# Products of 64 rows in two row tiles, layer 2 eleven units behind, and the split of x moved to ScalarE and GpSimd

## The reference, cut to what matters

```python
# x (2, 4096, 192), weight (8 heads, 7 taps)
w = softmax(weight)                          # over the taps
x = causal_convolution(x, w)                 # 7 taps, one set for 24 channels; 8192 tokens of 192
h = x @ w_in1                                # 192 -> 2048
P = a[0] + a[1]*h + a[2]*h*h + a[3]*h*h*h
Q = 1.0 + abs(b[0])*abs(h) + abs(b[1])*h*h
x = (P / (Q + 1e-6)) @ w_out1                # 2048 -> 192
h = x @ w_in2                                # 192 -> 2048
return (s * maximum(h, 0)**2 + b2) @ w_out2  # 2048 -> 192
```

## Time and profile before

| | us |
|---|---|
| median of 3 runs | 1260.81 (1260.74 to 1261.53) |
| the profiled execution, its own time | 1262.06 |
| its span, first to last instruction | 1260.3 |
| PE busy in the span | 1250.0 |
| DVE busy | 1118.3 |
| ACT busy | 1073.5 |
| POOL busy | 327.9 |

### The profile page before, as it was taken

How to read it: one execution, slowest core, us unless ns; L and a number is a source line. 1 busy time by engine, 2 the same in 40 slices (tenths; PEclk the granted TensorE clock), 3 DMA queues, 4 the chain that set the end, 5 groups by cost and what they waited for, 6 DMA issues and landing times.

```text
span 1260.3 us, 16271 instructions
## 1 busy us (share of the span) xinstructions
PE 1250.0 (99%) x6018; PEld 1078.5 (86%) x6018; DVE 1118.3 (89%) x1029; ACT 1073.5 (85%) x1093; POOL 327.9 (26%) x152
## 2 busy tenths in 40 slices
PE   8999999999999999999999999999999999999999
PEld 5768888888888888888888888888888888888888
DVE  7998999998999989998999989999899998889750
ACT  6998888888889898898888889898898888888853
POOL 3443222223223223222222222222222232232200
PEclk9999999999999999999999999999999999999999
DMA  8100000010000100000000100001000000000000
GB/s 230 56 13 13 1 14 1 5 34 0 12 0 12 25 0 12 0 12 25 12 0 0 38 0 12 0 0 38 0 12 0 12 0 1 13 1 13 1 13 13
DMA packets 14748, 20.39 MB, mean 16 GB/s; under 512 B 1792, under 2 KB 9984, under 8 KB 14592
## 3 DMA queue, kind: packets, MB, share of 16 engines
q1 hardware_dynamic: 14576, 20.01, 5.6%
q10 hardware_dynamic: 144, 0.01, 0.0%
HBM read 13.72 MB, written 6.29 MB: 16 GB/s over the span
## 4 chain that ended last, share of the span: by engine, by line
PE 97%; DMA 1%; DVE 0%; SPq 0%; ACT 0%; POOL 0%; issue 0%
PE o L466 26%; PE h L448 5%; PE h L449 5%; PE h L417 5%; PE o L438 5%; PE o_tail L439 5%; PE o_tail L432 5%; PE o L430 5%; PE o L431 5%; PE h L459 5%; PE h L453 5%; PE h L458 5%; PE h L418 5%; PE h L419 5%; PE h L420 5%; PE h L421 5%
## 5 line engine op out<-in xcount | busy, mean ns | idle before, releaser
L406 POOL TENSOR_TENSOR gl<-work,gh 128x1024 fp32r<-128x1024 f32 x126 | 304.6, 2418 | 819.8 <-ACT gh L690 812.9
L466 PE MATMUL o<-v,work 128*128 128x192 f32 x2048 | 353.2, 326 | 0.0
L466 PEld LDWEIGHTS o<-v,work 128*128 128x128 f32 x2048 | 339.2, 190 | 9.9
L680 ACT ACTIVATE work<-h,coef 128x1024 f32<-128x1024 f32 x128 | 154.3, 1206 | 136.2 <-PE h L421 134.7
L899 DVE SCALAR_TENSOR_TENSOR work<-work,coef,h 128x1024 f32<-128x1024 f32 x128 | 163.8, 1280 | 73.2 <-ACT work L681 70.5
L938 DVE SCALAR_TENSOR_TENSOR work<-work,coef 128x1024 f32<-128x1024 f32 x128 | 164.5, 1285 | 4.5
L905 DVE SCALAR_TENSOR_TENSOR work<-work,coef,h 128x1024 f32<-128x1024 f32 x128 | 164.0, 1281 | 4.5
L927 DVE SCALAR_TENSOR_TENSOR work<-work,coef 128x1024 f32<-128x1024 f32 x128 | 163.8, 1279 | 1.0 <-ACT work L685 1.0
L934 DVE SCALAR_TENSOR_TENSOR work<-work 128x1024 f32<-128x1024 f32 x128 | 156.8, 1225 | 4.4
L902 DVE TENSOR_TENSOR work<-work,h 128x1024 f32<-128x1024 f32 x128 | 155.5, 1215 | 0.0
L732 ACT ACTIVATE work<-h 128x1024 f32<-128x1024 f32 x128 | 130.1, 1017 | 23.9 <-PE h L459 23.9
(11 more groups left out here) (106 smaller groups left out, 2017.9 us busy)
## 6 DMA issues: line engine op xcount, KB each, us to landing
out_dram<-y_out SPq DMA_DIRECT2D x32, 192.0 KB, 2.0
xt<-in_x_main_dram SPq DMA_DIRECT2D x7, 518.0 KB, 5.2
xt_tail<-in_x_tail_dram SPq DMA_DIRECT2D x8, 259.0 KB, 5.4
work<-in_moe_w_out_dram SPq DMA_DIRECT2D x2, 768.0 KB, 9.2
v<-in_moe_w_out_dram SPq DMA_DIRECT2D x1, 1536.0 KB, 6.4
raw_w_tail_late<-in_moe_w_in_dram SPq DMA_DIRECT2D x4, 256.0 KB, 7.4
work<-in_moe_w_in_dram SPq DMA_DIRECT2D x2, 512.0 KB, 7.5
xt<-in_x_main_dram SPq DMA_DIRECT2D x2, 259.0 KB, 7.5
```

The source lines that it names most:

```text
L406: nc.gpsimd.tensor_tensor(gl[:, j % 2, :], r_buf[j % 2], gh[:, j % 2, :].bitcast(F32), ALU.subtract).then_inc(gl_ready, 1)
L466: return pe.matmul(o2[:, c // 2, c % 2, 0:D], g, v2[:, f, :], start=(f == 0 and c % 2 == 0), stop=(f == FT - 1), skip_group_check=True)
```

## The change

From tile 2 to tile 15 each PE unit is `unit_by_rows`: each product of 128 rows becomes two of 64 rows, one on partitions 0 to 63 and one on 64 to 127, issued in turn so that two neighbours have different rows and different PSUM banks. The products of the low tail by the low weights are dropped: this leaves 56 products of 64 rows by 512 columns (28 pairs) and 16 f32 ones of 192 columns (two records each, so 16 steps if two run at once) a unit. Where a bank turns from one row tile to the other, PE waits on a semaphore of its own (`h1_turned`, `h2_turned`, `o1_turned`, `o2_turned`). Part of the second product of layer 1 now stands inside the first one, so it waits for gh and gl early in the unit. `SKEW` goes from 10 to 11, `OUT1_LAG` from 2 to 3, `OUT2_LAG` from 1 to 2; the start (units 0 to 10) keeps its form by `EARLY`. `split_conv` is gone from DVE: ACT makes the high parts and POOL the low parts, at four steps of a pair, for pair i+1 at (1, 5) and (1, 7) and for the second batch of pair i at (0, 0) and (0, 1). Relu moves one step later, ahead of L680; the taps are at other steps.

```diff
-    SKEW = 10
-    OUT1_LAG = 2
-    OUT2_LAG = 1
+    SKEW = 11
+    OUT1_LAG = 3
+    OUT2_LAG = 2
+
+    EARLY = 10
...
-    TAPS_AT = {(0, 3): (("pair", 0), ("tail", 0)), (0, 4): (("pair", 1), ("tail", 1)), (0, 5): (("pair", 2), ("tail", 2)),
-               (0, 6): (("pair", 3), ("tail", 3)), (0, 7): (("pair", 4), ("tail", 4)),
-               (1, 0): (("pair", 5), ("tail", 5)), (1, 3): (("pair", 6), ("tail", 6))}
+    TAPS_AT = {(0, 1): (("pair", 0), ("tail", 0)), (0, 3): (("pair", 1),), (0, 5): (("pair", 2), ("tail", 1)),
+               (0, 6): (("pair", 3),), (0, 7): (("pair", 4), ("tail", 2)), (1, 0): (("pair", 5),),
+               (1, 1): (("pair", 6), ("tail", 3)), (1, 3): (("tail", 4), ("tail", 5)), (1, 5): (("tail", 6),)}
...
+    A_MAIN, A_TAIL = (1, 5), (1, 7)
+    B_MAIN, B_TAIL = (0, 0), (0, 1)
...
+        LOWER, UPPER = slice(0, P // 2), slice(P // 2, P)
...
+        def by_rows(t):
+
+            return not isinstance(t, int) or 2 <= t < TILES
+
+        def later_pair(i):
+            return not isinstance(i, int) or i > 0
```

On POOL, in step n, ahead of gl of unit n-2:

```diff
+            def low_of_x(pair, batch, n):
+                pool.wait_ge(x1_hi_ready, counted(pair * 4 + 2 * batch + 1))
+                pool.wait_ge(g_ready, counted(n))
+                nc.gpsimd.tensor_tensor(x1_lo[batch][:, :], conv[:, batch, :], x1_hi[batch][:, :].bitcast(F32),
+                                        ALU.subtract).then_inc(x1_lo_ready, 1)
...
+                    if tile(t) and pair_exists(i + 1) and (parity, j) == A_MAIN:
+                        low_of_x(i + 1, 0, n)
+                    if tile(t) and pair_exists(i + 1) and (parity, j) == A_TAIL:
+                        pool.wait_ge(x1_tail_copied, counted(i + 1))
+                        pool.wait_ge(g_ready, counted(n))
+                        rows = x1_tail[0][LOWER, :]
+                        nc.gpsimd.tensor_tensor(rows, conv_tail[LOWER, :], rows.bitcast(F32),
+                                                ALU.subtract).then_inc(x1_lo_ready, 1)
+                    if tile(t) and later_pair(i) and (parity, j) == B_MAIN:
+                        low_of_x(i, 1, n)
+                    if tile(t) and later_pair(i) and (parity, j) == B_TAIL:
+
+                        pool.wait_ge(x1_hi_ready, counted(i * 4 + 4))
+                        pool.wait_ge(gl_ready, counted(n - 2))
+                        pool.wait_ge(x1_lo_ready, counted(i * 4 + 3))
+                        pool.wait_ge(g_ready, counted(n))
+                        nc.gpsimd.tensor_tensor(x1_tail[1][LOWER, :], conv_tail[UPPER, :],
+                                                x1_tail[1][UPPER, :].bitcast(F32), ALU.subtract).then_inc(x1_lo_ready, 1)
+                        pool.wait_ge(x1_lo_ready, counted(i * 4 + 4))
```

On PE, the first part of `unit_by_rows` (`first_1`, `main_of_second_1` and `tail_of_second_1` issue one product of 64 rows each):

```diff
+                pe.wait_ge(t3_done, counted(n))
+                for at in range(4):
+                    last = first_1(0, False, at)
+                    if at == 3:
+                        last.then_inc(h1_turned, 1)
+                    last = first_1(1, True, at)
+
+                if k != 0:
+                    pe.wait_ge(out1_done, counted(n - OUT1_LAG))
+                    pe.wait_ge(gh_ready, counted(n - OUT1_LAG + 1))
+                    pe.wait_ge(gl_ready, counted(n - OUT1_LAG + 1))
+                    main_of_second_1(False, 0)
+                first_1(1, True, 4).then_inc(h1_turned, 1)
+                if k != 0:
+                    main_of_second_1(False, 1)
+                    tail_of_second_1(True, 0)
+                    main_of_second_1(False, 2)
+                pe.wait_ge(h1_turned, counted(since * 2 + 1))
+                first_1(0, True, 0)
+                pe.wait_ge(h1_turned, counted(since * 2 + 2))
+                for at in range(4):
+                    first_1(1, False, at)
+                    last = first_1(0, True, at + 1)
+                last.then_inc(h1_ready, 1)
```

After this it does the first half of the second product of layer 2 (`second_2(0)`), three pairs of the first product of layer 2, three pairs of the second of layer 1, `second_2(1)`, and the rest of both. On ACT and DVE:

```diff
+                    if unit(m - 1):
+                        act.wait_ge(h2_ready, counted(m))
+                        act.wait_ge(g2_ready, counted(m - 1))
+                        nc.scalar.activation(u_relu, h2_flat, ACT.Relu).then_inc(u_ready, 1)
+                    if tile(t) and pair_exists(i + 1) and (parity, j) == A_MAIN:
+                        convolved(i + 1)
+                        act.wait_ge(h1_ready, counted((i + 1) * 2 * UNITS - UNITS))
+                        nc.scalar.copy(x1_hi[0][:, :], conv[:, 0, :]).then_inc(x1_hi_ready, 1)
+                    if tile(t) and pair_exists(i + 1) and (parity, j) == A_TAIL:
+                        tail_convolved(i + 1)
+                        nc.scalar.copy(x1_tail[0][LOWER, :], conv_tail[LOWER, :]).then_inc(x1_tail_copied, 1)
+                    if tile(t) and later_pair(i) and (parity, j) == B_MAIN:
+                        act.wait_ge(h1_ready, counted(i * 2 * UNITS))
+                        nc.scalar.copy(x1_hi[1][:, :], conv[:, 1, :]).then_inc(x1_hi_ready, 1)
+                    if tile(t) and later_pair(i) and (parity, j) == B_TAIL:
+                        nc.scalar.copy(x1_tail[1][UPPER, :], conv_tail[UPPER, :]).then_inc(x1_hi_ready, 1)
...
-                    if tile(t) and pair_exists(i + 1) and (parity, j) == at(i, SPLIT_A, SPLIT_A_FIRST):
-                        split_conv(i + 1, 0)
-                    if tile(t) and pair_exists(i + 1) and (parity, j) == SPLIT_B:
-                        split_conv(i + 1, 1)
```

More of the change, by code:

```diff
@@ L62, in conv_rational_relu2_kernel @@
                7: (("pair_b", (3, 4, 5, 6)),), 8: (("tail", (0, 1, 2)),), 9: (("tail", (3, 4, 5, 6)),)}
-    SPLIT_A, SPLIT_A_FIRST = (1, 5), (1, 6)
-    SPLIT_B = (1, 7)
+    A_MAIN, A_TAIL = (1, 5), (1, 7)
+    B_MAIN, B_TAIL = (0, 0), (0, 1)
     FIRST_SECOND_SPLIT = 3
-    def at(i, usual, start):
-        return start if isinstance(i, int) and i == 0 else usual
     def pair_exists(i):
@@ L198, in conv_rational_relu2_kernel @@
         y_ready_out = sem("y_ready_out")
-        x1_tail_second = sem("x1_tail_second")
+        x1_tail_second, x1_tail_copied = sem("x1_tail_second"), sem("x1_tail_copied")
+        h1_turned, h2_turned = sem("h1_turned"), sem("h2_turned")
+        o1_turned, o2_turned = sem("o1_turned"), sem("o2_turned")
         W2_HALF = [slice(0, FF // 2), slice(FF // 2, FF)]
@@ L221, in in_h2 @@
         def in_h2(n):
-            return isinstance(n, int) and n < SKEW and n % 2 == 1
+            return isinstance(n, int) and n < EARLY and n % 2 == 1
         def is_unit_1(n):
@@ L229, in ahead @@
         def ahead(n):
-            return isinstance(n, int) and 1 <= n <= SKEW
+            return isinstance(n, int) and 1 <= n <= EARLY
         def cast_early(n):
-            return isinstance(n, int) and 0 <= n <= SKEW - 3
+            return isinstance(n, int) and 0 <= n <= EARLY - 3
         def late_exponential(n):
-            return not isinstance(n, int) or n >= SKEW - 1
+            return not isinstance(n, int) or n >= EARLY - 1
         def by_vector(n):
             return isinstance(n, int) and n >= NU - 2
+        def by_rows(t):
+            return not isinstance(t, int) or 2 <= t < TILES
+        def later_pair(i):
+            return not isinstance(i, int) or i > 0
         def is_end(n):
@@ L252, in tile, with is_last @@
             return not isinstance(t, int) or 0 <= t < TILES
+        def is_last(t):
+            return isinstance(t, int) and t == TILES - 1
         def first(t):
@@ L548, in product_of_layer_1 @@
                     pe.wait_ge(w_lo_ready, low)
-                two_buffers = isinstance(n, int) and n <= SKEW
+                two_buffers = isinstance(n, int) and n <= EARLY
                 pe.wait_ge(t3_done, counted(n - 1 if two_buffers else n))
@@ L581, in phase @@
                     t2 = t + (j - SKEW) // UNITS
-                    early = isinstance(n, int) and n < SKEW
-                    if unit(n) and not (isinstance(n, int) and n <= SKEW):
+                    if by_rows(t):
+                        unit_by_rows(n, j, t, parity, m, k2, t2)
+                        continue
+                    early = isinstance(n, int) and n < EARLY
+                    if unit(n) and not (isinstance(n, int) and n <= EARLY):
                         product_of_layer_1(n, j, t, parity)
@@ L690, in high_of_g, with convolved, tail_convolved @@
                 nc.scalar.copy(gh[:, buf, :], r_buf[buf]).then_inc(gh_ready, 1)
+            def convolved(pair):
+                if isinstance(pair, int) and pair == 1:
+                    act.wait_ge(conv_copied, 3)
+                else:
+                    act.wait_ge(main_step, counted(main_steps(pair)))
+            def tail_convolved(pair):
+                if isinstance(pair, int) and pair == 1:
+                    act.wait_ge(conv_copied, 3)
+                else:
+                    act.wait_ge(tail_step, counted(tail_steps(pair)))
             def phase(n0, t, i, parity):
@@ L728, in phase @@
                         nc.scalar.activation(q_buf[buf], q_buf[buf], ACT.Abs).then_inc(q_ready, 1)
```

(10 more changed lines are left out.)

93 lines of the change are left out of this document (92 added, 1 removed).

## The result

The kernel after takes 1475.89 us (median of 4 runs, 1475.84 to 1477.08), the one before 1261.04 (4 runs). The ratio is 1.1706, 95% interval 1.1685 to 1.1726: slower by 17%. The forecast was 1467, with a range of 1408 to 1562.

The account below looks back on a forecast made before the run. PE was taken to bound the kernel, with a loop nearly as long behind it. From 1262.06 us, -50.4 + 25 + 208 + 6 + 13 + 5 = +206.6 gave 1468.7, so a median of 1467; range 1408 to 1562.

Parts of the forecast that it names:

- POOL's wait is the loss: POOL's new low parts wait for g at n, holding up gl: 28 late steps, 26 at 8.0 us excess, 208 us.
- The two in the old form: Late steps at units 13 and 15, with PE's old products: excess 6.5 us each, 13 us.
- Row tiles run at once: PE: a pair of half products takes 0.227 us, so a unit takes 8.97 us, 50.4 us back over 112 units.
- The serial rival: PE: the two row tiles don't run at once, 17.9 us a unit, some 2225 us in all; chance 0.08.
- weight loads as a bound: PE: f32 steps at 0.20 us; the dear-pairs case, 0.65 to 0.8 on 86 units, 1523 to 1536 us.
- The clock: PE after a stall runs at the lower clock: late-step excess 8.0 us instead of 6.8, plus 6 us in following units.
- DVE's excess in a step with two taps: DVE: main plus tail tap take 2.00 us against 1.46 of room, 0.54 over, three times in a pair.
- The x2 split step: DVE: the x2 split takes 2.48 us, 1.02 over the room, 14 times.
- The units behind a late step: PE ends the unit late where no late step follows: 0.45 us more, 13 times, 6 us.
- The ends: Start and drain of the kernel: more PE work in the drain, less at the start, +5 us.
- The low end of the range: 1408 us: full clock (1430), pairs at 0.216 (10 less), and 10 for DVE's excesses.
- the rival without the stall: POOL's wait for g_ready doesn't stall, leaving -50.4 + 25 + 5: 1241 us; chance 0.04.

Follow-up runs that it names:

- experiment 1: Kernel after, with POOL's four new low parts waiting for g_ready at n-1 instead of n: 1260.59 us against 1261.19, ratio 0.9989.
- experiment 5: Kernel after, with POOL's wait at n-1 only at (0, 0) and (0, 1), still n at (1, 5) and (1, 7): 1357.75 us, one run.
- experiment 6: Kernel before, with only POOL's wait for g_ready at n added ahead of gl, no new operation: 1496.51 us against 1261.59.
- The run that kept PE busy: Kernel after, late waits kept, PE doing 7 products of zeros of 128 rows a stall before waiting for gl: 1446.41 us.
- experiment 2: Kernel after with POOL's wait at n-1 and PE's program written out for all 18 tiles, no hardware loop: 1246.74 us, ratio 0.9889.
- with the taps spread: Tail taps moved to steps with room, on experiment 1 (1260.80 us) and on experiment 2 (1245.79 us).
- experiment 8: Kernel after, POOL's wait still at n, with PE's program written out instead of looped: 1474.91 us, ratio 1.1693.
- The kept-busy runs: Kernel after with PE doing products of zeros before its wait for gl: 6 a stall on 64 rows, 1462.34 us; 7 of 128 rows, 1446.41 us.

## Why the prediction was right

*POOL's wait is the loss: right.* There are 28 late steps, 26 and 2, and the chain runs in the order given: g, low part, gl, then the logarithm and, but for the steps at (1, 7), PE. The 26 late steps of the row form last 17.00 us on the mean, forecast 17.0. By place they are 17.44 at (1, 5), 16.44 at (1, 7), 16.99 and 17.12 at (0, 0) and (0, 1). At (1, 5) it is 0.44 more than forecast: there the low part takes 1.70 us in all six late steps of the loop, beside a tail tap of DVE (L1004, 665.41), and 1.26 to 1.27 in the other eight places of L374, where no tap runs beside it; why isn't shown. At (1, 7) it is 0.56 less: where a tile starts on PE it waits for the low part of x first (a hole of 5.0 us and not 6 to 7, and it doesn't end with gl), does its four pairs while gl is made, and has its pitch of 0.23 back (at 698.9 in the tile behind the step shown) before h1 is done. The forecast knew neither, so that the mean came out at 17.0 is in part luck. The two in the old form last 15.6 and 16.7; with the unit between them they take 13.5 us more than in the kernel before, forecast 13. Experiments 1, 5 and 6 bear out the cause from three sides.

*Row tiles run at once: right.* The unit is 9.03 us where nothing else binds, forecast 8.97. The serial rival (17.9) is out, and so are weight loads as a bound. Half of the f32 product of a unit on PE, 16 records in 8 steps, and what starts behind it:

```profile
599.88 1.46 PE L665 MATMUL o<-v,work 64*128 64x192 f32 x16
601.05 0.53 PE L643 MATMUL h<-x_hi,w_hi 64*128 64x512 f32 x2
```

Its last record starts 1.12 after its first (1.46 less 0.34, the mean of one record), seven steps of 0.16, each with two weight loads of 64 rows. The Trainium skill (TensorE: Matmul & The Clock Gate, LDWEIGHTS) has a load of 128 columns at 107 ns however many rows it has. That a step of two loads needs 0.213 was the prediction's own step: it holds only if the two run one after the other, and by the 0.16 of this trace, where they go to different row tiles, they don't.

*The clock: right in sum, not in its parts.* Forecast 26 x 1.2 + 6 = 37 us. The run that kept PE busy gave back 29.5 and lost 7.8 at the jumps of the loop, which makes 37. But a late step gives back 1.5 at (1, 5) and (0, 1) and only 0.7 at (0, 0), some 26 us in all where the forecast had 31, and the units behind them give back 10, where it had 6.

*Terms that were off.* DVE's excess in a step with two taps is 0.25 (9.28 against 9.03), not 0.54, because I took the end of L905 and not the start of the next operation, which overlap by 0.08, and the unit was 0.06 longer; the rest is that the 2.00 for two taps came from a step which DVE doesn't bound, and in the kernel after they take 1.86 (1.20 + 0.66). The x2 split step lasts 9.90 as against 9.99 in the forecast. The units behind a late step cost more than the 6 us I gave them: against experiment 2 the six at (1, 6) take 4.9 us more, the seven at (0, 2), which hold the x2 split, 2.0, and the ones behind these at (0, 3) another 3. The ends cost 8 and not 5: 11.2 more behind the last step, where I had 7.2, and 3.2 less ahead of unit 13. The low end of the range should have been 1410 by its own terms. Without the stall (experiment 2) units 16 to 126 take 22.2 us less than before, where the forecast had 25.4. In the kernel after they add up to 1236.8 us against 1044.4, so +192.4 where the sum had +188.6; with 13.5 and 7.9 that is the 213.8 between the spans.

*What I did not see,* though it changed nothing here, is the jump back of PE's loop, 13.9 us in five jumps (1260.59 against 1246.74) and 15.0 with the taps spread. It lay hidden under the stall (experiment 8). It would have made the rival without the stall wrong: I gave it 1241, and it measured 1260.6 with the loop and 1246.7 without.

## What to carry to other kernels

When work is put into an in-order queue, write down for each of its waits when the awaited value is made, and what already stands behind it in that queue; a count that is one unit too late costs nothing in code and 8 us a time here, as the new operation waits and the old one behind it is the one that others need. Read a stall with the clock: PE came back from its holes of 5 to 7 us at 0.50 of it, and this second bill was a sixth of the whole (37 of 214 us). And after taking out a stall, look at the same place again, for what it had covered. Last, ask of two products at once what work they leave out: here a pair was worth one full product, and the gain was the four half products left out.

## What the runs showed of the hardware that I had not expected

A loop body of 16 units with 88 matmul records a unit (56 + 32) leaves PE idle for 1.86 to 2.30 us at each of its five jumps back (experiment 1); a body with 46 records a unit does not, and neither does the larger program written out, though its instruction queue moves 85 packets against 18. With the slow clock behind it a jump costs up to 3.4 us (12.92 against 9.57 in the same step of experiment 2), without it 1.6 to 2.0 (11.13 and 11.57).

The length of a pause alone doesn't settle whether PE comes back slow. Behind pauses of 1.5 us at (1, 5) the products started at the lower level in six of six steps, with products of zeros on 64 rows ahead of them, behind the 1.2 us at (0, 0) of the same run in two of seven, behind the 2 us at the jumps of experiment 1 in three of five, and behind 0.5 us, with products of 128 rows ahead of it, in none of six. The kept-busy runs differ both in the pause and in the rows, so which of the two decided isn't settled.
